# A fused attention and two-MLP kernel: sums of x, splits and last projections of the second MLP in another order

## The chip, the cores and the metric

The kernel runs on one core of a Trainium2 chip. The metric is the device time of one execution in microseconds, as the median of several runs. The engines are TensorE (PE, with its weight loads PEld), VectorE (DVE), ScalarE (ACT), GpSimd (POOL) and SyncE (SP), which here only issues DMAs, from its queue SPq.

## The reference

Three stages in float32, each working on the output of the one before:

```
attention: 4 batches, 8 heads, 576 positions, 64 wide; query i sees keys i-63..i
x  = attention output, 2304 tokens x 512
first MLP:   xn = x / sqrt(mean(x^2) + 1e-6) * rms_g
             x2 = (silu(xn @ w_gate) * (xn @ w_val)) @ w_out        # 512 -> 1536 -> 512
second MLP:  h  = x2 @ w_in                                         # 512 -> 2048
             out = (h * sigmoid(1.702 h)) @ w_out2                  # 2048 -> 512
```

## The kernel before, in words

**Split products.** Every matmul operand is split into a high part (a cast to the type fp32r) and a low part (the value less its high part). ScalarE or GpSimd makes the high part, VectorE the low part by a subtraction, and TensorE runs three matmuls per product: high x high, low weight x high, high weight x low (L657 to L659 in the first MLP, L789, L791, L793 and L850 to L852 in the second).

**First MLP.** Five tiles of tokens (t=0 to 4, the last four of 512), and for each twelve chunks of 128 hidden units (c=0 to 11). TensorE's order in a chunk is gate, val, then the projection of chunk c-2 (project_A); the attention steps of the next tile lie in between. Projections 10 and 11 of tile 4 are not in that loop: they are written by hand into the first pair of the second MLP. evacuate_A copies the four banks of a tile's result out, two on ScalarE (L1020) and two on VectorE (L1257), and SyncE stores them to x2_scratch in HBM.

**Second MLP.** Three blocks of 768 tokens (j=0 to 2), and in each eight pairs of hidden chunks (p=0 to 7), so 24 pairs, g=8j+p. Each pair is a 2 x 2 block product (512 inputs in two halves, 768 tokens in two halves of 384, 256 hidden units in two chunks) done with seven products in place of eight: P1, P6, P2, P7, P5, P4, P3, in this order, on two banks (BANK_A, BANK_B). It needs four sums of weights per pair (combine_w2 on GpSimd) and four sums of x per block of tokens: T1, T2, T3 (combine_x2) and T4 (last_x2_sum), on GpSimd. The seven x blocks B11, B21, B22, T1, T2, T3, T4 are each split once per j (xcB_hi_block on ScalarE, L949; xcB_lo_block on VectorE, L1168). VectorE puts the products together: two sums u (make_u, L1299), and C22, C21, C12 (make_c, L1305); ScalarE takes the sigmoid (L1072), VectorE multiplies (L1311), and the hidden block is split again (L1082, L1317).

**What sets the order.** Each engine runs a list written out by hand, and semaphores carry the data between them. In pair g TensorE runs P1, P6, P2, P7, the first six of twelve steps of the out projection of pair g-1 (out_B, 18 matmuls of 512), P5, P4, P3, then the other six. For g=0 there is no pair before; projections 10 and 11 stand between its products:

```
product_1(0); product_6(0); project_A(4, 10); product_2(0); project_A(4, 11, part 0)
product_7(0); project_A(4, 11, parts 1-3); product_5(0); product_4(0); product_3(0)
```

P3 waits for C22 of its pair (cB_made), P1 of the next pair for C12 (product_1, L797), P2 for ScalarE's copy of P1 (save_s1, L1061), P4 for both sums u. VectorE's list in a pair is: u2, low parts of w2in for pair g+1 (L1174), hidden C11, low part of w2out's first half (w2out_lo, L1180), u3, low part of hidden C11, w2out's second half, one x block for the next j when p > 0, then C22, hidden C22, C21, and so on to the low part of C12. ScalarE's list has the high parts in the same places (w2in_hi L961, w2out_hi L970). For j=0 the x blocks are split at c=5 to 11 of tile 4, w2in of pair 0 at c=9 and of pair 1 at c=11 and in pair 0.

**The loads.** SyncE's queue is one list too: after tile 3 it loads x2raw for j=0 and weight units 0 to 3; then x2raw for j=1; then it waits for all evacuations of tile 4 and stores them (store_x2, L391); and only behind that, for g=1, it loads the unit that holds w2out of pair 1 (load_w2, L383, 512 KB) and w2in of pair 3. Weights of the second MLP pass through three places in wstage.

## Time and profile before

| What | us |
|---|---|
| Median of 3 runs (919.36 to 919.68) | 919.51 |
| Time of the profiled execution | 919.45 |
| Its span (first to last instruction) | 917.7 |
| TensorE busy in the span | 897.0 (98%) |
| VectorE busy | 530.3 (58%) |
| ScalarE busy | 397.0 (43%) |
| GpSimd busy | 199.2 (22%) |

The span lies inside the profiled execution's time; the difference is start and end. A matmul counts as busy from its start to its modelled end, and the next one starts before that end, so a run of matmuls is read by the steps between their starts. The chain of work that ended last runs over TensorE for 94% of the span and over VectorE for 3%. The first MLP ends near 520 us; the second takes the rest.

### The profile page before, as it was taken

How to read it: one execution, taken by the hardware profiler on the slowest of the kernel's cores; microseconds unless marked ns; L12 is line 12 of the kernel's file. 1: busy time of each engine (PE TensorE's matmuls, PEld its weight loads, DVE VectorE, ACT ScalarE, POOL GpSimd, SP SyncE). 2: the span in 40 equal slices, each digit the busy share in tenths (PEclk: the TensorE clock that was granted, in tenths of full speed). 3: DMA queues.
4: the chain of work that ended last, by engine and by line, in shares of the span. 5: the costliest groups of instructions: out<-in, count | busy, mean ns of one | idle time of the engine just before them, and what ended most of it. 6: DMA issues, size and time to landing. Idle time of an engine off the chain costs nothing.

```text
span 917.7 us, 14688 instructions
## 1 busy us (share of the span) xinstructions
PE 897.0 (98%) x5372; PEld 772.5 (84%) x5372; DVE 530.3 (58%) x1143; ACT 397.0 (43%) x937; POOL 199.2 (22%) x222
## 2 busy tenths in 40 slices
PE   8799999999999999999999979999999999999998
PEld 7799888888888888888888868989878898999997
DVE  6896533334333343433334487777788777776754
ACT  5666233343333433433113344545445454545442
POOL 6234001120011201112202151231423132231300
PEclk9999999999999999999999989999999999999999
DMA  7672111201112101202200231121432212141201
GB/s 254 203 220 81 50 50 50 72 20 53 50 54 68 46 27 50 73 1 70 115 0 1 92 115 69 55 84 47 161 115 70 69 57 82 47 161 46 70 24 69
DMA packets 41079, 69.77 MB, mean 76 GB/s; under 512 B 3632, under 2 KB 13872, under 8 KB 41008
## 3 DMA queue, kind: packets, MB, share of 16 engines
q1 hardware_dynamic: 39600, 67.12, 22.5%
q10 hardware_dynamic: 1408, 1.70, 0.5%
q8 instruction: 44, 0.72, 0.3%
q14 instruction: 27, 0.22, 0.1%
HBM read 59.38 MB, written 9.44 MB: 75 GB/s over the span
## 4 chain that ended last, share of the span: by engine, by line
PE 94%; DVE 3%; ACT 2%; issue 1%; ACTq 0%
PE ps L657 16%; PE ps L659 15%; PE ps L658 15%; PE ps L851 7%; PE ps L852 7%; PE ps L850 7%; PE ps L789 7%; PE ps L793 6%; PE ps L791 6%; PE ps L642 2%; PE ps L614 2%; PE ps L628 2%; DVE w_all L1189 1%; PE ps L654 0%; ACT prob L894 0%
## 5 line engine op out<-in xcount | busy, mean ns | idle before, releaser
L657 PE MATMUL ps<-x_hi,w_all 128*128 128x512 f32 (+1 forms) x480 | 181.1, 377 | 0.2 <-DVE x_lo L1155 0.2
L659 PE MATMUL ps<-x_lo,w_all 128*128 128x512 f32 (+1 forms) x480 | 176.8, 368 | 0.0
L658 PE MATMUL ps<-x_hi,w_all 128*128 128x512 f32 (+1 forms) x480 | 176.7, 368 | 0.0
L852 PE MATMUL ps<-w2out,hB 128*128 128x512 f32 x288 | 112.9, 392 | 0.0
L851 PE MATMUL ps<-w2out,hB 128*128 128x512 f32 x288 | 112.9, 392 | 0.0
L850 PE MATMUL ps<-w2out,hB 128*128 128x512 f32 x288 | 112.0, 389 | 0.0
L657 PEld LDWEIGHTS ps<-x_hi,w_all 128*128 128x128 f32 x480 | 90.4, 188 | 19.3 <-issue 3.9
L658 PEld LDWEIGHTS ps<-x_hi,w_all 128*128 128x128 f32 x480 | 90.5, 188 | 15.4 <-issue 1.0
L659 PEld LDWEIGHTS ps<-x_lo,w_all 128*128 128x128 f32 x480 | 90.4, 188 | 15.3
L1227 DVE SCALAR_TENSOR_TENSOR sig<-sig,ps 128x512 f32<-128x512 f32 x48 | 32.9, 685 | 116.3 <-ACT sig L1004 116.3
L657 PE MATMUL ps<-h_hi,w_all 128*128 128x512 f32 (+1 forms) x240 | 89.8, 374 | 2.0 <-DVE hid L1236 1.9
L658 PE MATMUL ps<-h_hi,w_all 128*128 128x512 f32 (+1 forms) x240 | 88.4, 368 | 0.0
L659 PE MATMUL ps<-h_lo,w_all 128*128 128x512 f32 (+1 forms) x240 | 88.3, 368 | 0.0
L789 PE MATMUL ps<-xcB_even,w2in 128*128 128x384 f32 x224 | 77.3, 345 | 5.8 <-DVE u L1305 5.3
L1236 DVE TENSOR_TENSOR hid<-ps,sig 128x512 f32<-128x512 f32 (+1 forms) x60 | 38.3, 638 | 66.7 <-PE ps L659 53.0
L793 PE MATMUL ps<-xcB_even,w2in 128*128 128x384 f32 x224 | 76.4, 341 | 0.0
L791 PE MATMUL ps<-xcB_even,w2in 128*128 128x384 f32 x224 | 76.2, 340 | 0.0
L1014 ACT CAST h_hi<-hid 128x512 fp32r<-128x512 f32 (+1 forms) x60 | 34.8, 580 | 94.4 <-DVE hid L1236 94.3
L1004 ACT ACTIVATE sig<-ps 128x512 f32<-128x512 f32 x48 | 28.6, 597 | 106.4 <-PE ps L659 106.0
L523 POOL TENSOR_TENSOR wsum<-wstage 128x256 f32<-128x256 f32 x24 | 17.8, 741 | 259.1 <-DVE w2in L1174 259.1
L1072 ACT ACTIVATE sigB<-u 128x384 f32<-128x384 f32 x48 | 25.2, 525 | 107.5 <-DVE u L1305 107.5
L852 PEld LDWEIGHTS ps<-w2out,hB 128*128 128x128 f32 x288 | 54.0, 188 | 11.4
(138 smaller groups left out, 1721.3 us busy)
## 6 DMA issues: line engine op xcount, KB each, us to landing
wstage<-in_w_b SPq DMA_DIRECT2D x48, 512.0 KB, 3.5
wstage<-in_w_a SPq DMA_DIRECT2D x36, 256.0 KB, 3.1
vwin<-in_v_win SPq DMA_DIRECT2D x32, 256.0 KB, 3.7
kwin<-in_k_t SPq DMA_DIRECT2D x32, 160.0 KB, 3.4
x2raw<-x_scratch SPq DMA_DIRECT2D x3, 1536.0 KB, 6.9
out_dram<-yB SPq DMA_DIRECT2D x18, 256.0 KB, 4.3
qtok<-in_q_t SPq DMA_DIRECT2D x34, 128.0 KB, 2.6
x_scratch<-wstage SPq DMA_DIRECT2D x3, 1024.0 KB, 4.2
```

The costliest lines, as they stand in the source:

```text
L657: pe.matmul(out_, w[:, 0, cols], xh, start=first, stop=False, **flags)
L658: pe.matmul(out_, w[:, 1, cols], xh, start=False, stop=False, **flags)
L659: return pe.matmul(out_, w[:, 0, cols], xl, start=False, stop=last, **flags)
L789: pe.matmul(out_, w2in[:, g % 2, 0, a_, cols], x[:, b_, 0, d, :], start=fresh and d == 0, stop=False, skip_group_check=True)
L791: pe.matmul(out_, w2in[:, g % 2, 1, a_, cols], x[:, b_, 0, d, :], start=False, stop=False, skip_group_check=True)
L793: ins = pe.matmul(out_, w2in[:, g % 2, 0, a_, cols], x[:, b_, 1, d, :], start=False, stop=last, skip_group_check=True)
L850: pe.matmul(y, h[:, rows], w[:, 0, chunk, :], start=(p == 0 and first), stop=False)
L851: pe.matmul(y, h[:, rows], w[:, 1, chunk, :], start=False, stop=False)
L852: ins = pe.matmul(y, hB_of(g, chunk, 1)[:, rows], w[:, 0, chunk, :], start=False, stop=last)
L1014: nc.scalar.copy(h_hi[:, c % RING, 0:TILES_A[t][1]], hid[:, 0:TILES_A[t][1]]).then_inc(hidA_hi, 1)
L1227: nc.vector.scalar_tensor_tensor(out=sig[:, 0:w], in0=sig[:, 0:w], scalar=1.0, in1=gsc[:, :] if t == 0 else gate_of(t, c), op0=ALU.add, op ...
L1236: nc.vector.tensor_tensor(hid[:, 0:w], val_of(t, c), sig[:, 0:w], ALU.mult).then_inc(hidA_made, 1)
```

## The change

The four sums of x leave GpSimd (combine_x2 and last_x2_sum) and go to VectorE as sum_x2, one per pair, ahead of that pair's block: for j=1 and 2 in pairs p=1, 2, 3 and 5 in the order T1, T3, T2, T4, and for j=0 at c=4, 5, 6 and 8 of tile 4. The blocks of j=0 are split at c=4 to 10, w2in of pair 0 at c=7, of pair 1 at c=9, and w2out of pair 0 at c=11, where they stood later. Projection 10 is moved behind product 7 of pair 0 and projection 11 behind product 3; the evacuation of tile 4 goes with it, to ScalarE's place behind the sigmoid of C12 and VectorE's behind hidden C12. In every pair VectorE makes C12 ahead of the low part of C21. The semaphore waits are changed to suit, and one is added: in pair 0 hidden C11 waits for the last low part of the first MLP (hidA_lo).

```diff
--- before.py
+++ after.py
@@ -325,6 +325,11 @@
                 return x2_block(k)
             return {T1: x2sum(0), T2: x2sum(1), T3: x2raw[:, 0:KB, HB:TB], T4: x2sum(0)}[k]
 
+        SUM_ORDER = (T1, T3, T2, T4)
+
+        def sum_at(i):
+            return {0: T1, 1: T3, 2: T2, 4: T4}[i] if i in (0, 1, 2, 4) else None
+
         def x2stage(t):
             home = wstage if t < NA - 1 else late
             return home[:, 0:DC * TMAX].rearrange("p (c t) -> p c t", c=DC)
@@ -527,23 +532,6 @@
                 pool.wait_ge(w2_combined, done + 3)
                 nc.gpsimd.tensor_tensor(s4_, a12, s2_, ALU.subtract).then_inc(w2_combined, 1)
 
-            def combine_x2(j):
-                b11, b12 = x2raw[:, 0:KB, 0:HB], x2raw[:, 0:KB, HB:TB]
-                b22 = x2raw[:, KB:DC, HB:TB]
-                t1_, t2_, t3_ = (xcB_source(j, c) for c in (T1, T2, T3))
-                done = 4 * j
-                pool.wait_ge(x2_loaded, 16 * (j + 1))
-                nc.gpsimd.tensor_tensor(t1_, b12, b11, ALU.subtract).then_inc(x2_combined, 1)
-                pool.wait_ge(x2_combined, done + 1)
-                nc.gpsimd.tensor_tensor(t3_, b22, b12, ALU.subtract).then_inc(x2_combined, 1)
-                nc.gpsimd.tensor_tensor(t2_, b22, t1_, ALU.subtract).then_inc(x2_combined, 1)
-
-            def last_x2_sum(j):
-                pool.wait_ge(xcB_lo, COMBOS * j + T1 + 1)
-                pool.wait_ge(x2_combined, 4 * j + 3)
-                nc.gpsimd.tensor_tensor(xcB_source(j, T4), x2_block(B21), xcB_source(j, T2),
-                                        ALU.subtract).then_inc(x2_combined, 1)
-
             def scale_x(t, d):
                 n = TILES_A[t][1]
                 nc.gpsimd.tensor_tensor(xT[:, d, 0:n], xT[:, d, 0:n], rinv[:, 0:n], ALU.mult).then_inc(x_scaled, 1)
@@ -582,18 +570,11 @@
                         pool.wait_ge(rinv_ready, t + 2)
                         for d in range(DC):
                             scale_x(t + 1, d)
-            combine_x2(0)
-            last_x2_sum(0)
             combine_w2(0)
             combine_w2(1)
             for g in range(NP):
                 if g + 2 < NP:
                     combine_w2(g + 2)
-                if g % PB == 0 and g // PB + 1 < NB:
-                    combine_x2(g // PB + 1)
-                if g % PB == 5 and g // PB + 1 < NB:
-                    last_x2_sum(g // PB + 1)
-
         @block.tensor
         def _(pe):
             def scores(s):
@@ -857,14 +838,13 @@
 
             product_1(0)
             product_6(0)
+            product_2(0)
+            product_7(0)
             project_A(NA - 1, CA - 2)
-            product_2(0)
-            project_A(NA - 1, CA - 1, range(0, 1))
-            product_7(0)
-            project_A(NA - 1, CA - 1, range(1, DC))
             product_5(0)
             product_4(0)
             product_3(0)
+            project_A(NA - 1, CA - 1)
             for g in range(1, NP):
                 product_1(g)
                 product_6(g)
@@ -939,7 +919,7 @@
                 if k in (B11, B21, B22):
                     act.wait_ge(x2_loaded, 16 * (j + 1))
                 else:
-                    act.wait_ge(x2_combined, 4 * j + (4 if k == T4 else 3))
+                    act.wait_ge(x2_combined, 4 * j + SUM_ORDER.index(k) + 1)
                 if j == 0:
                     act.wait_ge(projA_done, (NA - 1) * CA + xcB_last_slot(k) + 1)
                 elif j == 1:
@@ -1042,12 +1022,13 @@
                     if t == 0 and c + 3 < CA:
                         weights_hi_by_act(c + 3, 0)
                         weights_hi_by_act(c + 3, 1)
-                    if t == NA - 1 and c >= CA - COMBOS:
-                        xcB_hi_block(0, c - CA + COMBOS)
-                    if t == NA - 1 and c == CA - 3:
-                        w2in_hi(0, range(IN_PIECES))
+                    if t == NA - 1 and 4 <= c < 4 + COMBOS:
+                        xcB_hi_block(0, c - 4)
+                    if t == NA - 1 and c in (7, 9):
+                        w2in_hi((c - 7) // 2, range(IN_PIECES))
                     if t == NA - 1 and c == CA - 1:
-                        w2in_hi(1, range(IN_PIECES))
+                        w2out_hi(0, 0)
+                        w2out_hi(0, 1)
                 if t < NA - 1:
                     act.wait_ge(val_done, CA * (t + 1))
                     split_x_hi(t + 1)
@@ -1094,11 +1075,11 @@
                 if g > 0 and g + 1 < NP:
                     w2in_hi(g + 1, range(IN_PIECES))
                 sigmoid_B(g, C11)
-                w2out_hi(g, 0)
+                if g > 0:
+                    w2out_hi(g, 0)
                 hid_hi_B(g, C11)
-                w2out_hi(g, 1)
-                if g == 0:
-                    evacuate_A(NA - 1)
+                if g > 0:
+                    w2out_hi(g, 1)
                 if p > 0 and j + 1 < NB:
                     xcB_hi_block(j + 1, p - 1)
                 sigmoid_B(g, C22)
@@ -1106,6 +1087,8 @@
                 sigmoid_B(g, C21)
                 hid_hi_B(g, C21)
                 sigmoid_B(g, C12)
+                if g == 0:
+                    evacuate_A(NA - 1)
                 if p == 0 and j > 0:
                     evacuate_y(j - 1)
                 hid_hi_B(g, C12)
@@ -1162,6 +1145,18 @@
                 nc.vector.scalar_tensor_tensor(out=x_lo[:, d, 0:n], in0=xT[:, d, 0:n],
                                                scalar=gcol[:, d:d + 1], in1=x_hi[:, d, 0:n].bitcast(F32),
                                                op0=ALU.mult, op1=ALU.subtract).then_inc(x_lo_ready, 1)
+
+            def sum_x2(j, k):
+                minuend, subtrahend = {T1: (x2raw[:, 0:KB, HB:TB], x2_block(B11)),
+                                       T3: (x2_block(B22), x2raw[:, 0:KB, HB:TB]),
+                                       T2: (x2_block(B22), x2sum(0)),
+                                       T4: (x2_block(B21), x2sum(1))}[k]
+                dve.wait_ge(x2_loaded, 16 * (j + 1))
+                wait(dve, x2_combined, 4 * j + SUM_ORDER.index(k))
+                if k == T4:
+                    dve.wait_ge(xcB_lo, COMBOS * j + T1 + 1)
+                nc.vector.tensor_tensor(xcB_source(j, k), minuend, subtrahend,
+                                        ALU.subtract).then_inc(x2_combined, 1)
 
             def xcB_lo_block(j, k):
                 dve.wait_ge(xcB_hi, COMBOS * j + k + 1)
@@ -1281,10 +1276,15 @@
                     hid_lo_A(t, c)
                     if split is not None:
                         weights_lo_A(split, 2)
-                    if t == NA - 1 and c >= CA - COMBOS:
-                        xcB_lo_block(0, c - CA + COMBOS)
-                    if t == NA - 1 and c == CA - 3:
-                        w2in_lo(0, range(IN_PIECES))
+                    if t == NA - 1 and 4 <= c < 4 + COMBOS:
+                        if sum_at(c - 4) is not None:
+                            sum_x2(0, sum_at(c - 4))
+                        xcB_lo_block(0, c - 4)
+                    if t == NA - 1 and c in (7, 9):
+                        w2in_lo((c - 7) // 2, range(IN_PIECES))
+                    if t == NA - 1 and c == CA - 1:
+                        w2out_lo(0, 0)
+                        w2out_lo(0, 1)
                 if t < NA - 1:
                     dve.wait_ge(val_done, CA * (t + 1))
                     for d in range(DC):
@@ -1306,6 +1306,8 @@
 
             def hidden_B(g, which):
                 dve.wait_ge(sigB_ready, 4 * g + which + 1)
+                if g == 0 and which == C11:
+                    dve.wait_ge(hidA_lo, CA * NA)
                 to = {C11: hid[:, 0:HB], C22: u3[:, :], C21: s1[:, :], C12: u2[:, :]}[which]
                 source = ps[:, BANK_A, 0:HB] if which == C11 else to
                 nc.vector.tensor_tensor(to, source, sigB[:, which % 2, :], ALU.mult).then_inc(hidB_made, 1)
@@ -1328,25 +1330,29 @@
             for g in range(NP):
                 j, p = divmod(g, PB)
                 make_u(g, u2, P6)
-                if g + 1 < NP:
+                if 0 < g < NP - 1:
                     w2in_lo(g + 1, range(IN_PIECES))
                 hidden_B(g, C11)
-                w2out_lo(g, 0)
+                if g > 0:
+                    w2out_lo(g, 0)
                 make_u(g, u3, P7)
                 hid_lo_B(g, C11)
-                w2out_lo(g, 1)
-                if g == 0:
-                    evacuate_A(NA - 1)
+                if g > 0:
+                    w2out_lo(g, 1)
                 if p > 0 and j + 1 < NB:
+                    if sum_at(p - 1) is not None:
+                        sum_x2(j + 1, sum_at(p - 1))
                     xcB_lo_block(j + 1, p - 1)
                 make_c(g, C22)
                 hidden_B(g, C22)
                 make_c(g, C21)
                 hid_lo_B(g, C22)
                 hidden_B(g, C21)
+                make_c(g, C12)
                 hid_lo_B(g, C21)
-                make_c(g, C12)
                 hidden_B(g, C12)
+                if g == 0:
+                    evacuate_A(NA - 1)
                 if p == 0 and j > 0:
                     evacuate_y(j - 1)
                 hid_lo_B(g, C12)
```

## Rows read from the trace of the kernel before

**Rows 1.** Waits of TensorE over the whole span: total us, times, longest.
```profile
PE ps L789 <- DVE u L1305: 7.0, 3, 4.2
```

**Rows 2.** Timeline of TensorE from 519 to 558: start us, us, engine, line, op.
```profile
519.78 0.39 PE L659 MATMUL ps<-h_lo,w_all 128*128 128x512 f32 x1
520.72 0.41 PE L789 MATMUL ps<-xcB_even,w2in 128*128 128x384 f32 x1 [0.55 <-issue]
...
532.48 0.34 PE L793 MATMUL ps<-xcB_even,w2in 128*128 128x384 f32 x1
533.85 0.44 PE L789 MATMUL ps<-xcB_even,w2in 128*128 128x384 f32 x1 [1.04 <-DVE u L1305]
...
534.84 0.34 PE L793 MATMUL ps<-xcB_even,w2in 128*128 128x384 f32 x1
539.41 0.66 PE L789 MATMUL ps<-xcB_even,w2in 128*128 128x384 f32 x1 [4.23 <-DVE u L1305]
...
545.30 0.34 PE L789 MATMUL ps<-xcB_even,w2in 128*128 128x384 f32 x1
...
557.75 0.33 PE L789 MATMUL ps<-xcB_even,w2in 128*128 128x384 f32 x1
```

**Rows 3.** Timeline of TensorE, pair 2: out projection, product 5, product 3.
```profile
561.93 0.39 PE L850 MATMUL ps<-w2out,hB 128*128 128x512 f32 x1
...
566.05 0.33 PE L789 MATMUL ps<-xcB_even,w2in 128*128 128x384 f32 x1
...
568.27 0.44 PE L789 MATMUL ps<-xcB_even,w2in 128*128 128x384 f32 x1
```

**Rows 4.** Windows, 538.50 to 538.75: PE, PEld, DVE, ACT, POOL, clock, DMA, GB/s.
```profile
538.50:538.75 0.25, 0.00 (x0) 0.00 (x0) 0.25 (x2) 0.00 (x0) 0.00 (x0) 0.50 1.15 377
```

**Rows 5.** Timeline of VectorE, pair 2: w2out, x block, C22, C21's low part, C12.
```profile
563.19 0.98 DVE L1180 TENSOR_TENSOR w2out<-wstage,w2out 128x512 fp32r<-128x512 f32 x1
...
566.26 1.49 DVE L1168 TENSOR_TENSOR xcB_odd<-x2raw,xcB_odd 128x768 fp32r<-128x768 f32 x1
567.67 0.54 DVE L1305 TENSOR_TENSOR u<-ps,u 128x384 f32<-128x384 f32 x1
...
571.56 0.56 DVE L1317 TENSOR_TENSOR hB<-s,hB 128x384 fp32r<-128x384 f32 x1 [0.58 <-ACT hB L1082]
572.04 0.55 DVE L1305 TENSOR_TENSOR u<-ps,u 128x384 f32<-128x384 f32 x1
```

**Rows 6.** Timeline of TensorE, from pair 8 to pair 9.
```profile
667.90 0.39 PE L852 MATMUL ps<-w2out,hB 128*128 128x512 f32 x1
670.02 0.41 PE L789 MATMUL ps<-xcB_odd,w2in 128*128 128x384 f32 x1 [1.73 <-DVE u L1305]
...
672.72 0.44 PE L789 MATMUL ps<-xcB_odd,w2in 128*128 128x384 f32 x1 [0.38 <-ACT s L1061]
```

**Rows 7.** Timeline of VectorE, pair 8, beside GpSimd's sums of x.
```profile
666.05 2.22 DVE L1311 TENSOR_TENSOR s<-s,sigB 128x384 f32<-128x384 f32 x1
```

**Rows 8.** Timeline of VectorE, first MLP, tile 4.
```profile
499.08 0.69 DVE L1227 SCALAR_TENSOR_TENSOR sig<-sig,ps 128x512 f32<-128x512 f32 x1 [2.94 <-ACT sig L1004]
...
503.34 0.96 DVE L1168 TENSOR_TENSOR xcB_even<-xT,xcB_even 128x768 fp32r<-128x768 f32 x1
```

**Rows 9.** Timeline of ScalarE, pair 1: w2out's first half.
```profile
545.89 0.61 ACT L970 CAST w2out<-wstage 128x512 fp32r<-128x512 f32 x1
```

**Rows 10.** Timeline of VectorE, pair 0: its two evacuations of tile 4.
```profile
532.06 1.28 DVE L1257 TENSOR_SCALAR late<-ps 128x512 f32<-128x512 f32 x2
```

**Rows 11.** Timeline of SyncE's queue: the store of tile 4.
```profile
533.41 0.37 SPq L391 DMA_DIRECT2D x_scratch<-late  x1
```

**Rows 12.** DMA issues from 533 to 534: KB each, median us to landing.
```profile
wstage<-in_w_b SPq DMA_DIRECT2D x1, 512.0 KB, 6.5
```

**Rows 13.** Timeline of GpSimd, pair 2: the last of its weight sums.
```profile
565.86 1.07 POOL L528 TENSOR_TENSOR wsum<-wstage,wsum 128x256 f32<-128x256 f32 x1
```

**Rows 14.** The page's part on DMA issues, whole span.
```profile
wstage<-in_w_b SPq DMA_DIRECT2D x48, 512.0 KB, 3.5
```

## The prediction, made before the change was run

> **What bounds the kernel now.** I read the list of TensorE's waits first, because TensorE is busy for nearly the whole span: whatever the change brings must come out of the few places where TensorE stands still, and whatever it costs must open new ones. In the second MLP only three waits on VectorE's sums L1305 are listed, 7.0 us together, the longest 4.2 [rows 1]. The timeline of TensorE then shows where they lie. In the first pair of feed-forward chunks (g=0) product 1 starts 0.94 us after the last matmul of the first MLP, where 0.23 is the normal step (18 matmuls of the out projection take 4.12 us [rows 2, 3]); product 3 starts 1.37 us after the one before it, and product 1 of g=1 starts 4.57 us after it [rows 2]. From there to 545.30 TensorE runs 18 matmuls in 5.89 us, 0.327 each; four products of g=2 (24 matmuls) take 4.18 us, 0.174 each [rows 2, 3]. So after that wait the clock is at the lower of its two levels, 1.2 GHz, and the profile's granted clock says so: 0.50 [rows 4].
>
> Second, the ordinary pair. In g=2 product 3 starts 2.22 us after product 5, where two products take 2.09; VectorE's sum C22, which product 3 needs, started 0.60 us earlier [rows 3, 5]. From the low part of w2out to C22 VectorE has no idle time [rows 5]. **So in pairs that also split a block of x, VectorE's chain already ends last**, by 0.1 us. Thirteen pairs show this same small step.
>
> Third, g=8: 2.12 us between two matmuls before product 1 and an idle 0.38 before product 2 [rows 6], while a VectorE operation is stretched to 2.22 us [rows 7] beside GpSimd's x sums.
>
> **The change part by part.** The sum is made on the profiled execution, 919.45 us (its span 917.7 and 1.75 around it); the median of the three runs is 0.06 above.
>
> *Blocks and weights sooner.* The seven x blocks move to c=4 to 10 and the two sets of w2in to c=7 and 9 of the first MLP. VectorE is idle 2.94 us per chunk there even with a block in it, and a further block-sized operation takes 0.96 there [rows 8], so nothing is added to TensorE's time. If this cover were gone, product 1 would wait as it does now. Gain: product 1 starts at 520.01, 0.71 sooner. ScalarE has two w2out casts (0.61 each, as in [rows 9]) where it had five casts, so the copy of s1 is ready before product 2.
>
> *Last projections.* Projection 10 now follows product 7 and projection 11 follows product 3. I walk TensorE with one product at 1.045 (a quarter of 4.18) and one projection chunk, 12 matmuls of 512, at 2.75 (12 x 0.229). Products 1, 6, 2, 7 end at 524.19, projection 10 at 526.94, products 5, 4, 3 at 530.08, projection 11 at 532.83. *C12 ahead of a low part:* in g=2 C12 starts 4.37 after C22, and 1.14 of that is the low part of C21 with its wait, 0.58 and 0.56 [rows 5]; without it 3.23. In g=0 C22 can start at 528.2, so C12 is done at 532.0, before 532.83: **the 4.57 us step, the 1.37 us step and the slow stretch all go.** In later pairs C12 is not what ends last (six out-projection steps, 4.12 us, lie over it), so there the move is worth nothing, and if that cover were gone it would be worth 1.1 a pair. The wait added for hid in g=0 is met by then.
>
> *What is late next.* Products 1 to 7 of g=1 end at 537.01, the out projection of g=0 at 541.13, products 5 and 4 at 543.22; there product 3 of g=1 could start. But the evacuation of the last first-MLP tile stays behind projection 11, and SyncE's queue holds the store of x2, then the load of w2out for g=1. Before, VectorE's two evacuations (1.28 us) began at 532.06 and the store was issued at 533.41 [rows 10, 11]. Now they come behind hidden C12 and projection 11: done about 534.3, store 534.35, load 534.8. **The load, issued 0.4 after the store, took 6.5 us to land before, because the 1 MB store is in front of it** [rows 12]; so it lands at 541.3. Before, ScalarE took this piece at 545.89 [rows 9] and nobody waited. Now ScalarE would be ready for it about 537.3. It stands 4 us, with hid C11's high part, w2out's second half and a block of x behind it; VectorE stands at the low part of w2out, with u3, hid C11, the sum, the block and C22 behind. ScalarE's cast ends at 541.9; from VectorE's low part to C22 it is 4.48 in g=2 [rows 5] and 0.88 more for the new sum: C22 at 547.3, product 3 at 547.9. A stall of 4.7 (about 0.9 of it already at product 4, which needs u3), plus 0.1 for the restart. Product 1 of g=2 then starts at 553.2 instead of 557.75: **this whole transition gains 4.6, not the 9.3 that it would without stalls.** A bound from below for the load is the same load with nothing ahead of it, as in the rivals.
>
> *x's sums on VectorE.* Pairs 1, 2, 3, 5 and 9, 10, 11, 13 each get one 768-element sum ahead of the block. Price: the block alone is 0.96 and its successor starts 0.08 before its end, so 0.88 [rows 8, 5]; a block that meets GpSimd is 1.49 long and takes 1.41 [rows 5]. Bounds 0.88 and 1.41. In g=2 GpSimd's last operation ends at 566.93 [rows 13], and the block's own work is the 0.82 left until 567.75 [rows 5]: it waited, then ran at full speed. The new sum takes that place and the wait with it, and the block behind runs alone. I take 0.88. Nothing hides it, since VectorE's chain ends last there. Seven pairs (the eighth is in the 4.7 above): **6.2 lost.** The Trainium skill, "SBUF — State Buffer", section "SBUF: two separate sides", says that VectorE and GpSimd hold their shared port pair exclusively for a whole instruction and the other is blocked. By it the sum and the block share one wait, 6.2; had they shared bandwidth, each sum would cost 1.41, 9.9 in all. The trace agrees, with the 0.82.
>
> *GpSimd without x sums.* At g=8 the step before product 1 shrinks from 2.12 to 0.23 (1.89) and the idle 0.38 with its restart goes (0.5); two more late steps of 0.1 to 0.2 beside it go too: 2.7 gained. VectorE's chain there, unstretched, has C12 at 665.9, over 2 us before product 1 wants it. The same sums at g=5 and 13 cost TensorE nothing now, and their going gives nothing. SyncE's later loads are issued no later relative to their pairs.
>
> Sum: 919.45 - 4.6 - 2.7 + 6.2 = **918.4**.
>
> **The rivals.**
> 1. *The clock falls in the new stall, and the change ends slower.* Before product 3 of g=1 TensorE would be idle 3.6 us, after 0.9 just before it. The old idle of 4.23, after 1.04, brought the clock down, but only at 538.5, with 0.9 of it left [rows 2, 4]; after the 1.73 at g=8 the next matmul is 0.41 long, as at 520.72, and not 0.66, as at 539.41 [rows 2, 6]. So the point lies between, and the new idle, 0.6 shorter than the old, would reach it, if at all, in its last 0.3; a load landing half a microsecond sooner keeps clear of it. Price: 18 matmuls took 5.89 instead of 3.13, so 2.8 to 3.1, giving 921.4. For it: 3.6 is nearer 4.23 than 1.73. Against: the margin is a tenth of the stall, and one fall in one trace does not say that a like idle always brings one; I take it at half the chance of the forecast.
> 2. *The load comes in time.* The same kind of load with nothing before it takes 3.5 [rows 14]. Then C22 is at 544.3, the stall 1.8, the time 915.4. Against: the row of this very load says 6.5 [rows 12].
> 3. *The sums cost the contended price,* 1.41 in all eight: 0.53 x 8 = 4.2 more, 922.6. For it only that both operations could meet GpSimd, if its sums shift later in the pair.
> 4. *The sums are hidden,* TensorE pays nothing: 7.0 less, 911.4. It would need idle time on VectorE ahead of C22, and there is none [rows 5].
>
> **How the numbers follow.** Forecast 0.50 (918.4, its own range 917.3 to 919.6: half a microsecond for the landing, 0.1 x 7 for the sums, 0.3 for the walk). Rival 1: 0.25, rival 2: 0.11, rival 3: 0.08, rival 4: 0.06. A measurement of this kernel can tell 0.2% from no change, so 917.7 and 921.3 are the limits. Faster: rivals 2 and 4 and a fifth of the forecast, 0.27. Slower: rival 3 and 0.6 of rival 1, 0.23. The rest, 0.50, within. The range 914.9 to 922.2 reaches over rivals 1 and 2 and leaves out rival 4, most of rival 3 and tails, under 2 in 10.
>
> **What would show it.** Right: product 1 of g=1 follows projection 11 with no wait; ScalarE waits about 4 us for a DMA into wstage before w2out's cast in g=1; product 3 of g=1 waits; in pairs 2, 3, 5, 9, 10, 11, 13 product 3 waits about 1 us for C22, and in 4, 6, 7 as now; no wait at product 1 of g=9. The granted clock at 548 decides rival 1. Wrong: w2out landed before ScalarE asks; product 3 in those pairs steps by 0.3; product 1 waiting in g=1; or waits inside the first MLP.

## The result, and the profile after

The changed kernel takes 921.44 us (median of 13 runs, 920.53 to 923.09), the kernel before 919.36 (13 runs beside them, 918.72 to 920.79): a ratio of 1.0022, 95% interval 1.0014 to 1.0031. It is 2.1 us slower. The forecast was 918.4, so its sign is wrong. What came is the mechanism of rival 1 (the clock falls in the new stall); that its 921.4 is also the time is luck, as the part on the prediction shows. The profiled execution of the changed kernel took 922.5 us, its span is 920.6.

The page's first part, engine by engine (busy us, share of the span, instructions), and the first line of its fourth, the chain that ended last:

```profile
PE 898.5 (98%) x5372; PEld 775.0 (84%) x5372; DVE 529.7 (58%) x1155; ACT 396.2 (43%) x937; POOL 173.6 (19%) x210
...
PE 87%; DVE 8%; issue 2%; DMA 1%; ACT 1%; ACTq 0%; SPq 0%; DVEq 0%
```

GpSimd has lost the sums (199.2 before); VectorE's total has hardly moved: the twelve sums it took over take 15.7 us, and other rows are shorter, the low parts of the x blocks by 3.8 in all, the hidden products by 3.8 and the low parts of w2out by 2.2. That this is because they meet fewer of GpSimd's rows is argued, not shown. Totals tell nothing of the 2 us, and the chain says only that TensorE is 87% of it. TensorE's waits do (total us, times, longest):

```profile
PE ps L770 <- DVE u L1305: 9.5, 8, 3.9
...
PE ps L770 <- DVE u L1299: 0.9, 1, 0.9
```

This answers to [rows 1]. Three waits of 7.0 have become eight of 9.5 and one of 0.9. They are one large stall in pair 1 (0.88 and 3.86) and seven small ones of 0.8. The timeline of TensorE shows the first (start us, us, engine, line, operation, idle before it); it answers to [rows 2]:

```profile
521.98 0.39 PE L640 MATMUL ps<-h_lo,w_all 128*128 128x512 f32 x1
522.21 0.33 PE L770 MATMUL ps<-xcB_even,w2in 128*128 128x384 f32 x1
...
534.84 0.39 PE L640 MATMUL ps<-h_lo,w_all 128*128 128x512 f32 x1
535.06 0.33 PE L770 MATMUL ps<-xcB_even,w2in 128*128 128x384 f32 x1
...
545.47 0.44 PE L770 MATMUL ps<-xcB_even,w2in 128*128 128x384 f32 x1 [0.88 <-DVE u L1299]
...
550.65 0.69 PE L770 MATMUL ps<-xcB_even,w2in 128*128 128x384 f32 x1 [3.86 <-DVE u L1305]
...
553.95 0.40 PE L831 MATMUL ps<-w2out,hB 128*128 128x512 f32 x1
...
568.75 0.45 PE L770 MATMUL ps<-xcB_even,w2in 128*128 128x384 f32 x1 [0.81 <-DVE u L1305]
```

Product 1 now follows the first MLP at once, and in pair 1 it follows projection 11 at once (535.06). Product 4 and product 3 of pair 1 then stand, and the nine matmuls from 550.65 to 553.95 take 3.30 us. At the pace of [rows 2, 3] the six products and three out-projection matmuls would take 6 x 0.174 + 3 x 0.229 = 1.73. The windows around the end of the stall (PE, PEld, DVE, ACT, POOL busy, granted clock, DMA share, GB/s), which answer to [rows 4]:

```profile
550.25:550.50 0.25, 0.00 (x0) 0.00 (x0) 0.25 (x1) 0.00 (x0) 0.00 (x0) 0.92 0.41 156
550.50:550.75 0.25, 0.10 (x1) 0.10 (x1) 0.09 (x1) 0.12 (x1) 0.00 (x0) 0.50 0.05 16
```

In this profile the clock fell to 1.2 GHz at the very end of the idle time, where the prediction had put it if at all; in two further profiles of the same kernel it fell elsewhere (below). What VectorE waited for is one chain: the store issued by SyncE's queue, the cast of w2out on ScalarE that waited for a DMA, then VectorE's own row, the new sum, the block and C22:

```profile
536.64 0.37 SPq L396 DMA_DIRECT2D x_scratch<-late  x1
```

```profile
543.60 0.62 ACT L950 CAST w2out<-wstage 128x512 fp32r<-128x512 f32 x1 [4.54 <-DMA wstage<-in_w_b]
```

```profile
544.26 0.69 DVE L1175 TENSOR_TENSOR w2out<-wstage,w2out 128x512 fp32r<-128x512 f32 x1 [3.67 <-ACT w2out L950]
...
547.26 1.47 DVE L1158 TENSOR_TENSOR xT<-x2raw 128x768 f32<-128x768 f32 x1
548.65 1.47 DVE L1163 TENSOR_TENSOR xcB_odd<-x2raw,xcB_odd 128x768 fp32r<-128x768 f32 x1
550.05 0.54 DVE L1305 TENSOR_TENSOR u<-ps,u 128x384 f32<-128x384 f32 x1
...
565.87 1.49 DVE L1158 TENSOR_TENSOR x2raw<-x2raw 128x768 f32<-128x768 f32 x1
567.28 0.94 DVE L1163 TENSOR_TENSOR xcB_odd<-x2raw,xcB_odd 128x768 fp32r<-128x768 f32 x1
568.15 0.54 DVE L1305 TENSOR_TENSOR u<-ps,u 128x384 f32<-128x384 f32 x1
```

The last three rows are an ordinary pair and answer to [rows 5]: the sum stands where the block stood and takes its wait (1.49), the block behind it runs alone (0.94). In pair 1 both are long (1.47): GpSimd's weight sums of that pair began only at 545.05, right behind VectorE's late row of w2out, and were beside both:

```profile
545.05 0.73 POOL L528 TENSOR_TENSOR wsum<-wstage 128x256 f32<-128x256 f32 x1 [33.39 <-DVE w2out L1175]
```

### The profile page after: what moved, and what is told of

Read it like the earlier page. It is cut to its first block, busy times and chain, and to the rows that moved or that the text cites. A ratio compares the mean times of both kernels' runs of the same rounds, so it can differ in the third digit from the quotient of the medians.

```text
span 920.6 us, 14697 instructions
## 1 busy us (share of the span) xinstructions
PE 898.5 (98%) x5372; PEld 775.0 (84%) x5372; DVE 529.7 (58%) x1155; ACT 396.2 (43%) x937; POOL 173.6 (19%) x210
## 4 chain that ended last, share of the span: by engine, by line
PE 87%; DVE 8%; issue 2%; DMA 1%; ACT 1%; ACTq 0%; SPq 0%; DVEq 0%
PE ps L638 16%; PE ps L639 15%; PE ps L640 15%; PE ps L832 6%; PE ps L833 6%; PE ps L831 6%; PE ps L770 5%; PE ps L774 5%; PE ps L772 5%; PE ps L623 2%; PE ps L595 2%; PE ps L609 2%; DVE w2in L1169 1%; DVE xT L1158 1%; DVE w2out L1175 1%
```

## The experiments

Four theories of the 2.1 us were to be told apart. **Load**: w2out's load behind the store makes the stall of pair 1. **Sums**: one sum a pair ahead of C22 costs 0.87 seven times, and more in pair 1. **Clock**: the fall at the end of the stall is a cost of its own. **Chance**: the first MLP and the runs scatter by as much as is to be explained.

**The kernel before, once more.** No edit.

> The kernel before, run as one of the kernels. In the two profiles at hand the changed kernel enters the second MLP 2.2 us later than the one before (last matmul of the first MLP at 521.98 against 519.78), though nothing was changed up to there, and its clock fell at about 7 and at 39 us. Theory A (the start differs from execution to execution, in both kernels): runs of this kernel show mean clocks from 0.996 down to 0.992 and their times spread by 2 us with them; a mean of 0.996 is the one fall at 538 of its profile, less means an early fall. Theory B (the changed program itself starts later): every run here has a clock of 0.996 and a time within 0.5 us of 919.4.

Measured: 919.0 (11 runs) beside 919.6, ratio 0.9996 (0.9987 to 1.0005). The same waits, 7.0 in three, the longest 4.2; mean clock 0.994 in this profile and 0.996 in that of [rows 1], with no difference in time that goes with it. The first MLP ends at 519.63, so this run gives no sign of the later start of the changed kernel; neither theory's picture of the clock fits, since 0.994 and 0.996 are both common here. The slow stretch behind the 4.2 stall is not the same in each execution, though. Summing what its steps exceed the ordinary ones gives 2.7 us in the first profile, 2.1 here and 1.4 in a third (below), and the clock fell at 537.15 here, 2.1 before the end of the idle time, where it was 0.9 before it in the first profile:

```profile
537.00:537.25 0.25, 0.00 (x0) 0.00 (x0) 0.25 (x2) 0.00 (x0) 0.00 (x0) 0.80 0.92 197
```

**Load ahead of the store.** In SyncE's list:

```
             load_x2(1)
+            load_w2(out_unit(1))
             store_x2(NA - 1)
             for g in range(1, NP):
-                load_w2(out_unit(g))
+                if g > 1:
+                    load_w2(out_unit(g))
```

> The changed kernel with the load of pair 1's w2out issued ahead of the store of x2. Theory (the store in front of that load makes the stall of pair 1): ScalarE's 4.5 us wait for the DMA goes; product 3 of pair 1 waits 1.0 us as in the other pairs with a sum; the clock stays at 1.00 around 550; 3.9 us from the stalls (5.1 in steps now, 1.1 left) and 1.6 from the clock: 5.3 us faster than the changed kernel, 916.0. Rival (VectorE's list is the bound there, the load only happens to end with it): under 1 us faster.

Measured: 914.29 (5 runs), ratio 0.9943 (0.9931 to 0.9956): 5.3 us below before, and 7.4 below the changed kernel, each against the runs of before beside it. The whole stall of pair 1 is gone, and the clock stays at 2.4 GHz there. The load is now issued at 513.07, since it no longer waits for the evacuations of tile 4 either, and lands at 521.66, well before ScalarE casts it. So the run shows that the load's place in the queue makes the stall; how much of it is the later issue and how much the store's data in front is not told apart by it. Its waits of TensorE, and VectorE's rows in pair 1:

```profile
PE ps L772 <- DVE u L1307: 5.7, 7, 0.8
```

```profile
540.60 0.96 DVE L1160 TENSOR_TENSOR xT<-x2raw 128x768 f32<-128x768 f32 x1
541.47 0.96 DVE L1165 TENSOR_TENSOR xcB_odd<-x2raw,xcB_odd 128x768 fp32r<-128x768 f32 x1
542.60 0.56 DVE L1307 TENSOR_TENSOR u<-ps,u 128x384 f32<-128x384 f32 x1 [0.17 <-PE ps L776]
```

More came back than the load's own share: GpSimd waits for its load until 541.20 here, so the sum and the block both run at 0.96, and C22 even waits for TensorE. In this one pair the sum is hidden. The seven waits of 0.8 stand, so they have nothing to do with the load.

**Sums to the end of VectorE's list.** The sum that was ahead of the block is done at the end of the pair before, behind the last low part:

```
                 if p > 0 and j + 1 < NB:
-                    if sum_at(p - 1) is not None:
-                        sum_x2(j + 1, sum_at(p - 1))
                     xcB_lo_block(j + 1, p - 1)
...
                 hid_lo_B(g, C12)
+                if j + 1 < NB and sum_at(p) is not None:
+                    sum_x2(j + 1, sum_at(p))
```

> The changed kernel with each sum of x at the end of VectorE's list of the pair before, where it waits 1.1 us for TensorE. Theory (each sum lengthens the chain to C22 by 0.88 us, which TensorE waits for): the seven 1.0 us waits at product 3 go back to 0.1, the stall of pair 1 is 0.9 to 1.4 shorter and with it, likely, the clock does not fall: 6.2 + 1.2 + 1.6 = 9 us faster than the changed kernel, 912.4; without the last two 915.2. Rival (the sum costs the pair wherever it stands, since VectorE is full): no more than 2 us faster.

Measured: 913.44 (5 runs), ratio 0.9935 (0.9922 to 0.9949), 6.2 below before. All seven steps are back at 0.11 over the ordinary one, as in the kernel before, and the wait at product 3 of pair 1 is 1.4 shorter. The rows of TensorE, and the windows around them:

```profile
544.71 0.34 PE L774 MATMUL ps<-xcB_even,w2in 128*128 128x384 f32 x1
547.52 0.44 PE L770 MATMUL ps<-xcB_even,w2in 128*128 128x384 f32 x1 [2.47 <-DVE u L1305]
...
548.04 0.52 PE L774 MATMUL ps<-xcB_even,w2in 128*128 128x384 f32 x1
```

```profile
547.75:548.00 0.25, 0.25 (x2) 0.25 (x2) 0.00 (x0) 0.25 (x1) 0.00 (x0) 0.75 1.01 393
548.00:549.00 1.00, 1.00 (x4) 1.00 (x4) 0.94 (x2) 0.37 (x2) 0.00 (x0) 0.50 0.39 141
```

After an idle time of 2.47 the clock fell all the same, 0.4 us after TensorE had gone on working, so the hope that it would not was wrong.

**Both.** The edits of the last two together.

> Both. If the two costs are apart from each other: 5.3 + 6.2 + 0.9 = 12.4 us faster than the changed kernel, 909.0. If the sum in pair 1 was hidden under the late load: 0.9 less of gain, 909.9. No wait over 0.3 us is left on TensorE in the second MLP.

Measured: 908.94 (4 runs), ratio 0.9882 (0.9869 to 0.9896). No wait of TensorE on VectorE's sums is listed in the second MLP. Load and sums explain all of the new stalls: from the last matmul of the first MLP to the last of all it is 382.5 us here, 388.3 with the load alone, 387.8 with the sums alone, 395.1 in the changed kernel.

**The changed kernel, once more.** No edit.

> The changed kernel again. From the last matmul of the first MLP to the end of the span its profile took 398.62 us against 397.92 for the one before, so 0.7 more; the medians differ by 2.1. Theory A (the late entry into the second MLP, 521.98, was a start of that one execution; the program itself enters as before): this profile enters at 519.6 to 520.5 and the median is 0.4 to 1.2 above the kernel before on the same chip. Theory B (the changed program enters later as a rule): entry again above 521 and a median 1.5 to 2.5 above.

Measured: 921.93 (6 runs) beside 919.3 (16 runs), ratio 1.0031 (1.0019 to 1.0042). The same waits: 9.5 in eight, the longest 3.9. Neither theory fits: the first MLP ends at 520.04, as theory A has it, and the median is 2.6 above the kernel before, which theory B had. Here the clock fell near the start of the stall, three microseconds before product 3 (548.74), and not at its end:

```profile
545.50:545.75 0.25, 0.00 (x0) 0.00 (x0) 0.25 (x1) 0.00 (x0) 0.25 (x1) 0.98 0.00 0
545.75:546.00 0.25, 0.00 (x0) 0.00 (x0) 0.25 (x1) 0.00 (x0) 0.25 (x1) 0.50 0.00 0
```

**C12 behind the low part again.** In VectorE's list:

```
-                make_c(g, C12)
                 hid_lo_B(g, C21)
+                make_c(g, C12)
```

> The changed kernel with C12 again behind the low part of C21 in every pair. Theory (worth nothing but in pair 0): C12 of pair 0 ends 1.15 us later, at 1.4 after projection 11 would have let product 1 start less 0.85 of slack, so product 1 of pair 1 waits 0.3 to 0.5 us and nothing else moves: 0.3 to 0.5 slower than the changed kernel. Rival (the later C12 is felt in every pair): 1 us or more slower.

Measured: 922.4 (4 runs) beside 919.3, ratio 1.0036 (1.0022 to 1.005). Its interval and that of the run before overlap, so the medians show no difference; the profiles do, 396.7 against 395.4 from the last matmul of the first MLP on. TensorE's rows in pair 1:

```profile
533.67 0.41 PE L770 MATMUL ps<-xcB_even,w2in 128*128 128x384 f32 x1 [0.28 <-DVE u L1305]
...
544.88 0.44 PE L770 MATMUL ps<-xcB_even,w2in 128*128 128x384 f32 x1 [1.40 <-DVE u L1299]
```

Product 1 waits 0.28 where it followed at once, so C12's place is needed there, by that much. The second row was not foreseen: VectorE's evacuations stand behind C12, so the store and the load behind it are later too, and the idle time before product 4 is 1.40 instead of 0.93. In the other pairs nothing differs: the prediction's "worth nothing" holds. In all the profile is 1.3 to 1.7 slower than those of the changed kernel, more than the 0.3 to 0.5 expected: 0.5 with the first row, 0.5 with the second, the rest mostly in the slow stretch.

**The stall filled.** TensorE gets 20 matmuls of 384 columns into a free bank between product 4 and product 3 of pair 1:

```
+                if g == 1:
+                    for _ in range(20):
+                        pe.matmul(ps[:, 5, 0:HB], w2in[:, 1, 0, A22, 0:P], xcB_even[:, T4, 0, 0, :],
+                                  start=True, stop=True)
```

> The changed kernel with 20 further matmuls of 384 columns (3.5 us, into a bank that nobody reads) between products 4 and 3 of pair 1, where TensorE waits 3.9 us; the output is untouched. Theory (the fall of the clock in that stall costs 1.6 us: nine matmuls took 3.3 us instead of 1.73): the granted clock stays 1.00 around 551, product 3 starts where it did, and the kernel is 1.6 us faster than the changed one. Rival (the fall costs nothing of its own, since VectorE's chain of the next pair sets the end): the same time.

Measured: 919.39 (11 runs) beside 919.3, ratio 1.0001 (0.9992 to 1.001): 2.5 below the changed kernel by the medians, 1.2 to 1.5 by the profiles (393.9 against 395.1, 395.4 and 395.1). Product 3 starts where it did in the stall:

```profile
549.01 0.44 PE L770 MATMUL ps<-xcB_even,w2in 128*128 128x384 f32 x1 [0.40 <-DVE u L1309]
```

```profile
549.00:553.00 4.00, 3.99 (x19) 3.49 (x20) 3.23 (x7) 2.50 (x5) 0.00 (x0) 1.00 0.00 0
```

The stall is as long as before the edit, only the clock is kept, at 1.00. So the fall is a cost of its own, and with it gone the change is worth nothing either way.

**The sums back on GpSimd.** The old two functions and their calls return (the last sum of j=0 now behind the first weight sums), and VectorE's two calls go; all else of the change stays:

```
+                if g % PB == 0 and g // PB + 1 < NB:
+                    combine_x2(g // PB + 1)
+                if g % PB == 5 and g // PB + 1 < NB:
+                    last_x2_sum(g // PB + 1)
...
-                    if sum_at(p - 1) is not None:
-                        sum_x2(j + 1, sum_at(p - 1))
```

> The changed kernel with the four sums of x back on GpSimd where they were, all else as changed. Theory (seven sums at 0.87 us on VectorE cost 6.1, GpSimd's sums stretch VectorE in pair 8 by 2.7, the stall of pair 1 loses 0.9): the waits at product 3 are back to 0.1, the 1.9 us step before product 1 of pair 9 is back: 4.3 us faster than the changed kernel, 917.1, and pair 0 perhaps 0.5 slower under GpSimd's sums. Rival (moving the sums was the useful part): slower than the changed kernel.

Measured: 915.75 (5 runs), ratio 0.9966 (0.9953 to 0.9978). Moving the sums was the part that lost: 6.2 by the medians, 5.4 to 5.7 by the profiles. What they cost on GpSimd at the change of halves, now that C12 is sooner, is the row before product 1 of pair 9; it answers to the 1.73 of [rows 6]:

```profile
665.87 0.41 PE L794 MATMUL ps<-xcB_odd,w2in 128*128 128x384 f32 x1 [0.57 <-DVE u L1327]
```

The steps there exceed the ordinary ones by 0.72 and 0.52, 1.2 together; in the kernel before it was 1.9 and 0.55, 2.4. The blocks-alone run below, which has GpSimd's sums too and C12 in its old place, keeps the 1.9. So 1.2 of the 2.7 that the prediction gave to the moved sums would have come from C12's new place alone.

**The best of both, and the block behind C22.** The edits of load and sums, and the low part of the block behind C22, where nothing of TensorE's waits for it:

```
+                make_c(g, C22)
                 if p > 0 and j + 1 < NB:
                     xcB_lo_block(j + 1, p - 1)
-                make_c(g, C22)
                 hidden_B(g, C22)
```

> The kernel of e4 (load first, sums at the end of the pair) with the low part of the x block moved behind C22 in VectorE's list. Theory (in the thirteen or so pairs with a block VectorE's chain to C22 is 0.1 us too long and the restart costs another 0.1, while from C22 to C12 there are over 1 us to spare): the steps of 0.28 us at product 3 go, 2.5 us faster than e4, 906.4. Rival (the block then delays C12 past product 1 of the next pair, or the next pair's u2 past product 7): new waits there, same time or slower.

Measured: 905.16 (5 runs) beside 919.36 (19 runs), ratio 0.9843 (0.983 to 0.9857). The small step before product 3, which the prediction had counted in thirteen pairs, is gone. VectorE now waits for TensorE before C22:

```profile
558.50 0.56 DVE L1307 TENSOR_TENSOR u<-ps,u 128x384 f32<-128x384 f32 x1 [0.99 <-PE ps L776]
558.97 0.95 DVE L1165 TENSOR_TENSOR xcB_odd<-x2raw,xcB_odd 128x768 fp32r<-128x768 f32 x1
```

It is the fastest kernel here, 14.2 us below before and 16.3 below the changed one.

**Blocks and weights sooner, alone.** In the kernel before, the seven x blocks go to c=4 to 10 and w2in to c=7 and 9 of the first MLP, on ScalarE and VectorE alike. With them come the changed kernel's wait at hidden C11 of pair 0, and on GpSimd the weight sums of pair 0 go ahead of the last sum of x; nothing else of the change:

```
-                    if t == NA - 1 and c >= CA - COMBOS:
-                        xcB_lo_block(0, c - CA + COMBOS)
+                    if t == NA - 1 and 4 <= c < 4 + COMBOS:
+                        xcB_lo_block(0, c - 4)
...
-                if g + 1 < NP:
+                if 0 < g < NP - 1:
                     w2in_lo(g + 1, range(IN_PIECES))
```

> The kernel before with only the x blocks of j=0 at c=4 to 10 and w2in of pairs 0 and 1 at c=7 and 9. Theory: product 1 of pair 0 starts 0.7 us sooner, nothing else is on the path, since the 1.4 and 4.6 us steps come from VectorE behind projection 11's evacuation and from C12: 0.7 faster than the kernel before. Rival (VectorE's freed 2 us in pair 0 bring C22 and C12 sooner too): 2 us or more faster. It also enters the second MLP with the first MLP's program unchanged: 519.6 to 519.8 if the entry goes with the execution, 520.0 to 520.5 if it goes with the changed lists.

Measured: 915.59 (5 runs), ratio 0.9952 (0.994 to 0.9965): 3.8 below before, where 0.7 was expected and "2 us or more" was the rival. Besides product 1's 0.8 the wait at 533.85 of [rows 2] is gone (1.3) and the one at 539.41 is 1.2 shorter. The split of w2in that left pair 0 was not on VectorE's path: before, VectorE stood idle for 1.34 behind it. But GpSimd's weight sums waited for that split and its sums of x stood behind them, so before they ran from 529.40 to 535.64, beside VectorE's rows of w2out and hidden C22. GpSimd's and VectorE's rows before:

```profile
529.40 2.19 POOL L536 TENSOR_TENSOR xT<-x2raw 128x768 f32<-128x768 f32 x1
```

```profile
529.78 2.36 DVE L1180 TENSOR_TENSOR w2out<-wstage,w2out 128x512 fp32r<-128x512 f32 x1
...
534.39 1.66 DVE L1311 TENSOR_TENSOR u<-u,sigB 128x384 f32<-128x384 f32 x1 [0.59 <-ACT sigB L1072]
```

With the split done sooner, GpSimd's sums run from 520.38 to 526.01, while VectorE waits anyway, and the two rows take 0.68 and 0.56:

```profile
520.38 1.87 POOL L536 TENSOR_TENSOR xT<-x2raw 128x768 f32<-128x768 f32 x1 [10.70 <-DMA x2raw<-x_scratch]
```

```profile
529.05 0.68 DVE L1178 TENSOR_TENSOR w2out<-wstage,w2out 128x512 fp32r<-128x512 f32 x1
```

That is 2.8 us less on VectorE on the way to C12 of pair 0. Rows of TensorE, and two windows:

```profile
536.33 0.41 PE L789 MATMUL ps<-xcB_even,w2in 128*128 128x384 f32 x1 [3.02 <-DVE u L1303]
...
537.55 0.52 PE L789 MATMUL ps<-xcB_even,w2in 128*128 128x384 f32 x1
```

```profile
536.00:537.00 1.00, 0.67 (x4) 0.70 (x5) 0.41 (x2) 0.53 (x1) 0.00 (x0) 1.00 0.99 326
537.00:538.00 1.00, 1.00 (x6) 1.00 (x5) 0.42 (x2) 0.64 (x2) 0.00 (x0) 0.65 1.05 406
```

The clock fell here too, a microsecond after TensorE had resumed.

**Before and after, a third time.** No edits.

> The kernel before once more, for the entry into the second MLP. Eight profiles of the changed lists entered at 519.95 to 520.53 (one at 521.98), two of the kernel before at 519.63 and 519.78. If the entry varies by execution alone, this one may be anywhere from 519.6 to 520.5; if it goes with the program, 519.6 to 519.8.

Measured: 919.13 (11 runs), ratio 1.0000 (0.9991 to 1.0008). The first MLP ends at 520.18: the start of the second differs from execution to execution in the kernel before too.

> The changed kernel once more, beside the kernel before as h3 on the same chip. Entry at 520.0 to 520.5 and 398.6 to 399.0 from there to the end of the span; the median 1.8 to 2.6 above the kernel before: 1.1 from the second MLP (1.6 of it the clock), 0.5 from the entry, 0.2 outside the span.

Measured: 921.6 (9 runs), ratio 1.0024 (1.0014 to 1.0033). The entry, at 520.84, lies outside the range; the second MLP and the median lie within. The three comparisons of the changed kernel agree: 1.0022, 1.0031, 1.0024. The first MLP ends at 519.63 to 520.18 in the three profiles of before, and at 521.98, 520.04 and 520.84 in those of the changed kernel. The last matmul comes 394.3, 393.9 and 393.3 after that in the one, 395.1, 395.4 and 395.1 in the other.

## Why the prediction was wrong, and where it was right

*Product 1 of g=0* (0.71): right, it starts one ordinary step after the last projection. *Product 1 of g=1 behind projection 11*: right. With the first MLP ending 2.20 later in the profile than in that of before, the walk gives 532.83 + 2.20 = 535.03; the row says 535.06.

*Store, load and ScalarE*: right. Forecast with the same shift 536.55, 543.5; measured 536.64, 543.60, with 4.54 of waiting for the DMA.

*The stall of pair 1*: sized 0.4 too small. The two steps lost 1.05 + 0.11 and 4.03, 5.2 us, where 4.8 were forecast. The prediction took 0.88 for the sum, because sum and block share one wait for GpSimd. They do in pair 2. In pair 1 both meet GpSimd, 1.47 each, and C22 came 0.5 later for it. That is rival 3's mechanism in one pair of eight, and its condition, GpSimd's sums later in the pair, is met there because they start right behind VectorE's own late row of w2out.

*The sums on VectorE* (6.2 for seven): right. The step before product 3 exceeds the ordinary one by 0.98 instead of 0.11 in pairs 2, 3, 5, 9, 10, 11 and 13, 7 x 0.87 = 6.1. Both experiments that take the sums from there gain it, and the part in pair 1 with it: 8.3 us with the sums moved on (6.2 below before, where the changed kernel is 2.1 above), and 6.2 with them on GpSimd (915.75 against 921.93), where pair 9 loses 1.2 again. The Trainium skill, "SBUF — State Buffer", section "SBUF: two separate sides", has VectorE and GpSimd hold the shared ports one after the other; this rule gave the 6.2, and shared bandwidth would have given 9.9. The measured 6.1 agrees with the rule.

*No wait at g=9* (2.7): right as a sum, but 1.2 of it belongs to C12's place. *Pairs 4, 6, 7*: right, as before.

**The step that failed is the forecast's term for the new stall:** it has the idle time alone and puts the fall of the clock in it at nothing. The reason given stands under rival 1: the point of the fall lies between an idle of 1.73 and one of 4.23, the new one "would reach it, if at all, in its last 0.3", and so the fall got half the chance of the forecast. It fell in all three profiles of the changed kernel, 0.2 before the end of the idle time, 3.0 before it, and 0.2 after TensorE had resumed:

```profile
549.25:549.50 0.25, 0.05 (x1) 0.05 (x1) 0.14 (x1) 0.07 (x1) 0.00 (x0) 1.00 0.00 0
549.50:549.75 0.25, 0.25 (x1) 0.25 (x2) 0.00 (x0) 0.25 (x1) 0.00 (x0) 0.79 0.00 0
```

It also fell with every other idle time of 2.44 us or more in these runs that was left unfilled: 3.88, 3.02, 2.47 and 2.44. The moment at which one trace showed it was no measure of how long an idle time must be.

What the fall costs is read from how much of the slow stretch TensorE works in. A step of 384 columns takes 0.320 there in place of 0.174, so 0.46 of that time is lost. In the three profiles of before TensorE worked 5.9, 4.7 and 3.0 us at 1.2 GHz and lost 2.7, 2.1 and 1.4; in those of the changed kernel 3.2, 3.8 and 3.4 and lost 1.5, 1.75 and 1.6. So rival 1's price of 2.8 to 3.1 was nearly twice too high, since it was taken from the longest stretch of three. The filled stall confirms the lower one, 1.2 to 1.5 by the profiles.

That corrects the other side too: the kernel before lost 2.1 on average where the prediction subtracted 2.7. By the profiles, from the end of the first MLP on, the sum then reads: forecast -1.1, with 0.6 less to gain from the old slow stretch, 1.6 for the new one, 0.4 to 0.5 for the longer stall, +1.6. The means of three profiles each say 395.17 - 393.83, +1.3. Without the clock's fall the change would have been worth nothing (the filled stall, ratio 1.0001), which is still 1 us short of the forecast: the 0.6 and the 0.4 to 0.5. That rival 1's 921.4 is the measured time is luck: its price was 1.4 too high, and against that stand the same 0.6 and 0.4 to 0.5, and some 0.7 from outside the second MLP, which no part of the prediction had.

**Left open.** Of the 2.1 us in the medians 1.3 lie in the second MLP. The rest is in the first MLP and outside the span. The changed kernel's first profile has waits of 1.1 and 0.7 on the first loads, seen in the two rows below, and the first MLP ended at 521.98; in the runs that differ from it only behind that point it ended at 519.95 to 520.53. All of this lies in the first 91 us: from the 901st matmul (at 90.77 in the kernel before) to the last one of the first MLP it is 428.98 to 429.05 us in all fourteen profiles. So the sums and blocks that moved into tile 4 cost TensorE nothing there, as forecast, and up to that matmul the engines' lists are the same in both kernels. The difference between executions is as large as that between the kernels, and no run here tells whether the changed program has a part in it.

```profile
PE ps L595 <- DMA rinv<-in_k_t: 1.1, 1, 1.1
...
PE ps L595 <- DMA hid<-in_k_t: 0.7, 1, 0.7
```

The move of the last projections was never tried alone, nor was the load ahead of the store in the kernel before. The nearest pair is the run with the sums on GpSimd and the one with the blocks alone: they differ by that move, C12's place and the early w2out of pair 0, and take 389.7 and 390.2. Since C12's place is worth 1.2 at pair 9, the move with the stall that it makes gained nothing; that is worked out from two profiles, not shown by a run of its own.

## What to carry to other kernels

Where the chain of a helping engine ends last, an operation ahead of the one that TensorE waits for costs nearly its full length in every iteration (0.87 of 0.96 here, nothing in the one pair with slack); behind it, or at the end of the list, the same operation was free (the sums' move gave 8.3 us, 1.6 of them in the stall of pair 1; the block's 3.5 by the medians, 2.9 by the profiles). When a large store is moved, look at what stands behind it in the same queue: a 512 KB load kept behind a late store of 1 MB made a stall of 5.2 us, and with the load first there was none. When an operation moves, look at what a third engine starts behind it: the split of w2in, itself off the path, had held GpSimd's sums at a place where they cost VectorE 2.8 us. Weigh a new stall of some microseconds on TensorE with the clock's fall in it, and take the price from several profiles, since one stall of the same kernel cost between 1.4 and 2.7.

## What the runs showed of the hardware that was not expected

The fall of the clock is not bound to the idle time itself. With idles of 4.2 it came 0.9, 2.1 and 0.4 before the end, with 3.85 up to 3.0 before it and up to 0.2 behind it, with 2.47 it came 0.4 us after TensorE had resumed and with 3.02 a full microsecond after, while TensorE was busy. The Trainium skill, "TensorE: Matmul & The Clock Gate", section "Part 1: The HAM clock gate", says that the activity monitor runs free of the kernel, so that the moment of a switch varies. These rows agree: neither the start of a slow stretch nor its cost (1.4 to 2.7 in three profiles of one kernel) can be read off the length of a stall.

Nor is there one length that divides the idle times with a fall from those without. The idle of 1.73 at g=8 brought no slow matmul in any profile of before. But among the first chunks of the first MLP an idle of 2.16 or 2.17 near 38 us stands in eleven of the fourteen profiles, and a slow stretch began within 1.4 us of its end in seven of them, not in the other four; and in the run with the load first one began 1.0 after an idle of 1.77:

```profile
29.93 0.36 PE L640 MATMUL ps<-h_hi,w_all 128*128 128x256 f32 x1 [1.77 <-DVE hid L1233]
```

```profile
31.00:32.00 1.00, 1.00 (x7) 1.00 (x6) 1.00 (x8) 0.27 (x1) 0.79 (x1) 0.50 0.75 172
```

So at about 2 us it is a matter of the execution; from 2.44 on it fell each time here, ten times in all.

The load of w2out behind the store took 6.5 us from issue to landing in the changed kernel too, as in [rows 12] and as forecast, against a median of 3.5 over the span [rows 14]. The store took 5.2, so the load landed 1.8 behind it; the load issued at 547.36, with no store near it, took 3.6. The rows of issues from 536.5 to 537.3 (KB each, median us to landing):

```profile
x_scratch<-late SPq DMA_DIRECT2D x1, 1024.0 KB, 5.2
wstage<-in_w_b SPq DMA_DIRECT2D x1, 512.0 KB, 6.5
```
